# An attention stage and two mixers on one core: the first supergroup by plain weights, and values in longer runs

## The reference, cut to what matters

```python
q_s, k_s = softmax(q, axis=-1), softmax(k, axis=tokens)       # over features; over tokens
x = einsum(q_s, einsum(k_s^T, v))                             # linear attention, (8, 576, 512)
u = x + (relu(x^T @ w_tok1) @ w_tok2)^T                       # token mixing, 576 -> 256 -> 576
y = u + relu(u @ w_ch1) @ w_ch2                               # first mixer,  512 -> 1536 -> 512
out = y + relu(norm(y) * g @ w_ch1') @ w_ch2'                 # second mixer, 512 -> 2048 -> 512
```

## Time and profile before

| | |
|---|---|
| median of 3 runs | 1565.05 us (1563.29 to 1566.54) |
| the profiled execution | 1563.69 us, its span 1561.9 us |
| attention stage | 0 to 243.5 us |
| first mixer, positions 0 to 4 | start at 243.5, 386.9, 501.4, 616.4, 730.0 us |
| second mixer, positions 5 to 9 | start at 844.3, 987.8, 1131.2, 1274.7, 1418.1 us |
| PE, DVE, ACT, POOL busy | 94%, 69%, 45%, 20% of the span |
| mean granted clock | 0.990 |

### The profile page before, as it was taken

How to read it: one execution, slowest core, us unless ns; L and a number is a source line. 1 busy time by engine, 2 the same in 40 slices (tenths; PEclk the granted TensorE clock), 3 DMA queues, 4 the chain that set the end, 5 groups by cost and what they waited for, 6 DMA issues and landing times.

```text
span 1561.9 us, 19837 instructions
## 1 busy us (share of the span) xinstructions
PE 1472.2 (94%) x7584; PEld 1322.4 (85%) x7584; DVE 1076.6 (69%) x1165; ACT 698.2 (45%) x844; POOL 309.0 (20%) x315
## 2 busy tenths in 40 slices
PE   6999896898999999899989999999999999999998
PEld 5988885787888887788878888888888888889998
DVE  7987876397486486496696687568657856872276
ACT  5656654352453453352452453344345424532342
POOL 6587785323303312300000000000000000000000
PEclk9999998899999999999999999999999999999999
DMA  7899985989989989979658767766876687667766
GB/s 241 256 306 296 299 282 202 403 318 366 354 291 379 372 294 362 352 288 317 240 184 300 248 209 266 249 247 219 275 243 228 237 277 244 211 219 256 251 214 199
DMA packets 150334, 429.28 MB, mean 275 GB/s; under 512 B 14240, under 2 KB 43488, under 8 KB 150240
## 3 DMA queue, kind: packets, MB, share of 16 engines
q1 hardware_dynamic: 132768, 361.94, 67.6%
q0 software_dynamic: 17472, 66.07, 11.8%
HBM read 348.26 MB, written 79.69 MB: 274 GB/s over the span
## 4 chain that ended last, share of the span: by engine, by line
PE 74%; DMA 10%; DVE 7%; issue 3%; SPq 2%; POOL 2%; ACT 2%; DVEq 0%; ACTq 0%; POOLq 0%
PE ps L1131 24%; PE ps L1133 23%; PE ps L1132 23%; DMA w_ring<-w_scratch_B 6%; DMA vt<-v 2%; SPq L289 2%; DMA qt<-q 1%; DVE o_lo L980 1%; DVE x_lo L834 1%; PE ps L1155 1%; DMA w_op<-w2b 1%; PE ps L1166 1%; DVE q_sum L761 1%; POOL q_lo L464 0%; DVE h L950 0%
## 5 line engine op out<-in xcount | busy, mean ns | idle before, releaser
L1131 PE MATMUL ps<-x_hi,w_ring 128*128 128x462 f32 (+1 forms) x980 | 369.2, 377 | 44.1 <-issue 15.1
L1131 PE MATMUL ps<-o_hi,w_ring 128*128 128x462 f32 (+1 forms) x980 | 367.4, 375 | 9.6 <-DVE o_lo L980 7.9
L1133 PE MATMUL ps<-x_hi,w_ring 128*128 128x462 f32 (+1 forms) x980 | 366.7, 374 | 0.0
L1132 PE MATMUL ps<-x_lo,w_ring 128*128 128x462 f32 (+1 forms) x980 | 366.7, 374 | 0.0
L1132 PE MATMUL ps<-o_lo,w_ring 128*128 128x462 f32 (+1 forms) x980 | 364.8, 372 | 0.0
L1133 PE MATMUL ps<-o_hi,w_ring 128*128 128x462 f32 (+1 forms) x980 | 364.6, 372 | 0.0
L671 ACT CAST o_hi<-h 128x924 fp32r<-128x924 f32 (+1 forms) x210 | 202.3, 963 | 254.8 <-PE ps L1133 225.0
L980 DVE TENSOR_TENSOR o_lo<-h,o_hi 128x924 fp32r<-128x924 f32 (+1 forms) x210 | 240.8, 1150 | 61.2 <-ACT o_hi L671 61.2
L1131 PEld LDWEIGHTS ps<-x_hi,w_ring 128*128 128x128 f32 x980 | 186.2, 190 | 74.3 <-issue 31.2
L1131 PEld LDWEIGHTS ps<-o_hi,w_ring 128*128 128x128 f32 x980 | 185.1, 189 | 40.1 <-issue 17.5
L950 DVE TENSOR_TENSOR h<-ps,h 128x924 f32<-128x924 f32 (+1 forms) x90 | 100.6, 1117 | 163.5 <-PE ps L1133 163.1
(11 more groups left out here) (140 smaller groups left out, 1831.3 us busy)
## 6 DMA issues: line engine op xcount, KB each, us to landing
w_ring<-w_scratch_C SPq DMA_DIRECT2D x280, 512.0 KB, 3.8
w_ring<-w_scratch_B SPq DMA_DIRECT2D x210, 512.0 KB, 5.6
w_scratch_C<-w_out POOLq DMA_DIRECT2D x8, 1792.0 KB, 11.7
w_scratch_C<-last_pair POOLq DMA_DIRECT2D x8, 1792.0 KB, 11.8
w_scratch_B<-w_out POOLq DMA_DIRECT2D x6, 1792.0 KB, 10.4
w_scratch_B<-last_pair POOLq DMA_DIRECT2D x6, 1792.0 KB, 9.9
kt<-kT SPq DMA_DIRECT2D x32, 288.0 KB, 6.0
u_scratch<-u_out SPq DMA_DIRECT2D x32, 288.0 KB, 3.8
```

Of the source, the lines that this page charges most:

```text
L1131: mm(dst, a_hi, b_hi, start=start, stop=False, skip_group_check=onto)
L1132: mm(dst, a_hi, b_lo, start=False, stop=False, skip_group_check=onto)
L1133: return mm(dst, a_lo, b_hi, start=False, stop=stop, skip_group_check=onto)
```

## The change

Position 0 is no longer a list of ring entries. Its products are plain: for each of 12 units of raw weights (6 of the first matrix, 6 of the second) PE does 48 matmuls of 462 columns, 576 in all, reading the raw blocks from SBUF: slots 0, 5 and 6 of `w_out`, and the fourth block in ring slot 3 (`plain_w`). `CALLS` begins with position 1. The 12 units are all made in this stage: the raw half of a unit first (`hi_raw` on ACT, `lo_raw` on DVE, three instructions each), then the four sums (`sum_unit`, `hi_sums`, `lo_sums`), and its store, which is read from position 1 on. In the attention stage only units 0 and 1 are loaded (batches 5 and 6). POOL makes no remainders of weights any more. `w_out` gets a second buffer of its own. x is split in four parts without sums (`plain_x`), and the hidden blocks in twelve (`hi_po`, `lo_po`). PSUM holds four groups of two banks, which ACT empties with a relu (`plain_take`) after every second unit of the first matrix; `plain_add` adds the last ones into `res`. SP loads x of position 1 and the residual right behind the attention stage, then three ring entries. Units of the second mixer are made at 5 entries in each of positions 1 to 3, unit 12 at the end of position 0.

`vt` becomes [128, 5, 2, 257]: 128 values, one, 128 values, so the ones of two neighbours share a column, and the host lays v out so that four fifths of a batch come in one DMA of runs of 1,024 bytes, with four small ones for the ends and the tail.

```diff
-                for t, rows in ST:
-                    sp.dma_start(vt[0:rows, t, :, 0:P], v[b, t * P:t * P + rows, :].rearrange("p (c e) -> p c e", c=NC))
+                full = vt[:, 0:NT - 1, :, :].rearrange("p t a w -> p (t a w)")
+                w, n = 2 * P + 1, (NT - 1) * NC // 2
+                src = v[b, 0:P * n * 2 * P].rearrange("(p x) -> p x", p=P)
+                sp.dma_start(full[:, P + 1:P + 1 + (n - 1) * w].rearrange("p (n w) -> p n w", w=w)[:, :, 0:2 * P],
+                             src[:, P:P + (n - 1) * 2 * P].rearrange("p (n w) -> p n w", w=2 * P)).then_inc(v_in, 16)
...
             step(NB - 1, 0)
             phase_a_over(sp)
+            for c in range(NC):
+                load_x(1, c)
+            for c in range(NC):
+                load_res(0, c)
+            for n in range(RW - 1):
+                load_entry(n)
+            for c in range(NC):
+                load_x(2, c)
+            store_plain(0)
+            store_plain(1)
+            load_entry(RW - 1)
+            store_plain(2)
+            store_plain(3)
...
-                load_unit(i)
+                if i in (NB - 3, NB - 2):
+                    load_unit(i - (NB - 3))
                 if later:
                     sub_q(i + 1, ST)
-                sum_unit(i - 1)
-                if later:
                     lo_q(i + 1)
-                lo_unit(i - 1)
-                store_unit(i - 1)
+                else:
+                    sum_unit(0)
+                    sum_unit(1)
...
+            for n in range(PLAIN):
+                if n >= 2:
+                    sum_unit(n)
+                store_unit(n)
+                load_unit(n + 2)
...
+            def hi_raw(n):
+                act.wait_ge(wp_in[n % 2], 32 * (n // 2 + 1))
+                wait(act, wp_stored[n % 2], 16 * (n // 2))
+                if n >= 2:
+                    act.wait_ge(groups, unit_over(n - 2))
+                x = w_op[:, n % 2, :, :]
+                nc.scalar.copy(w_out[n % 2][:, 0, 0, :], x[:, 0, :]).then_inc(raw_hi_made, 1)
+                nc.scalar.copy(plain_w(n, 0, 1)[:, 0, :], x[:, 7, :]).then_inc(raw_hi_made, 1)
+                nc.scalar.copy(w_out[n % 2][:, 5:7, 0, :], x[:, 5:7, :]).then_inc(raw_hi_made, 1)
...
+            def plain(n):                                   # ACT
+                if 2 <= n + 1 < PLAIN:
+                    hi_raw(n + 1)
+                if n < HC["B"]:
+                    if n % 2 == 1:
+                        plain_take(n, 0)
+                    hi_sums(n + 1)
+                    if n == 4:
+                        hi_po(0)
+                        hi_po(1)
+                    if n % 2 == 1:
+                        for g in range(1, NC):
+                            plain_take(n, g)
+                    return
...
                 else:                                       # DVE, batches 1 to 7
                     norm_kv(i)
-                    if later == 0:
-                        sum_x(0, 0)
...
+                if later == 0:
+                    lo_raw(1)
+                    lo_px(0)
+                    lo_px(1)
                 if first:
                     max_q(1, ST[3:])
...
+            def plain_in(n):                                # PE, units of the first matrix
+                pe.wait_ge(raw_lo_made, 3 * (n + 1))
+                if n == 0:
+                    pe.wait_ge(px_lo_made, NC)
+                for g in range(NC):
+                    if n == 0 and g == 1:
+                        pe.wait_ge(u_act, U_ACT * NB)
+                        pe.wait_ge(u_dve, U_DVE * NB)
+                    if n >= 2 and n % 2 == 0:
+                        pe.wait_ge(plain_relu, NC * (n // 2 - 1) + g + 1)
+                    for i in range(2):
+                        x = plain_product(plain_w(n, i, g // 2), g % 2, g, *plain_x(2 * i + n % 2),
+                                          n % 2 == 0 and i == 0, n % 2 == 1 and i == 1)
+                    x.then_inc(groups, 1)
```

More of the change, by code:

```diff
@@ L29, in mixer_kernel @@
     CONSTS = 10
+    V_LOADS = 5
     SIZES = [462, 462, 462, 462, 456]
@@ L52, in mixer_kernel @@
     entries = g2_entries = 0
-    for pos in range(NX):
+    for pos in range(1, NX):
         stage, sg = "BC"[pos // NSG], pos % NSG
@@ new lines, in hi_sums, with plain_take, hi_po @@
+            def hi_sums(n):
+                act.wait_ge(wp_sum, 4 * (n + 1))
+                nc.scalar.copy(w_out[n % 2][:, 1:5, 0, :], w_op[:, n % 2, 1:5, :]).then_inc(wp_hi, 1)
+            def plain_take(n, g):
+                act.wait_ge(groups, mixed(n, g))
+                nc.scalar.activation(plain_hidden(g // 2 * HC["B"] + n // 2 * 2 + g % 2), plain_group(g), ACT.Relu)\
+                  .then_inc(plain_relu, 1)
+            def hi_po(r):
+                if r >= RO:
+                    act.wait_ge(groups, added(r - RO))
+                nc.scalar.copy(o_hi[:, r % RO, :, 0:SIZES[0]], plain_hidden(r % 2 * HC["B"] + r // 2)).then_inc(po_hi_made, 1)
@@ L624, in step @@
                             hi_q(i + 1, ST[c - 1:c])
-                    if later == 0 and c == 0:
-                        hi_x(0, 1)
+                    if later == 0 and c < 2:
+                        hi_px(2 + c)
                 if later:
                     hi_q(i + 1, ST[3:])
-                if later and not first:
-                    hi_unit(i - 1)
+                if later == 1:
+                    hi_raw(0)
+                    hi_raw(1)
             exp_q(0, ST)
@@ L691, in norm @@
                       .then_inc(root_made, 1)
-            hi_unit(NB - 2)
-            for p in (2, 3):
-                hi_x(0, p)
-            hi_unit(NB - 1)
+            hi_sums(0)
+            for n in range(PLAIN):
+                plain(n)
             for c in CALLS:
@@ new lines, in plain_add, with plain @@
+            def plain_add(g):
+                n = SIZES[0]
+                y = halves(res, n)[:, g, :, :]
+                if g == 0:
+                    dve.wait_ge(res_in, 64)
+                dve.wait_ge(groups, added(2 * HC["B"] - 1, g))
+                nc.vector.tensor_tensor(y, plain_group(g), y, ALU.add).then_inc(plain_out, 1)
+            def plain(n):
+                if 2 <= n + 1 < PLAIN:
+                    lo_raw(n + 1)
+                if n == 4:
+                    lo_po(0)
+                    lo_po(1)
+                r = 2 * (n - HC["B"]) + 2
+                if 2 <= r < 2 * HC["B"]:
+                    lo_po(r)
+                if n + 1 < PLAIN:
+                    lo_sums(n + 1)
+                else:
+                    lo_unit(PLAIN, 0)
+                    lo_unit(PLAIN, 1)
+                if 2 <= r < 2 * HC["B"]:
+                    lo_po(r + 1)
+                if n == 6:
+                    sum_x(1, 0)
+                if n == 7:
+                    lo_x(1, 0)
+                    lo_x(1, 1)
+                    sum_x(1, 1)
+                if n == 8:
+                    lo_x(1, 2)
+                    sum_x(1, 2)
+                    lo_x(1, 3)
+                if n == 9:
+                    lo_x(1, 4)
+                    lo_x(1, 5)
+                    sum_x(1, 3)
+                if n == 10:
+                    lo_x(1, 6)
@@ L941, in _ @@
             nc.vector.tensor_scalar(g_half[:, :], gcol[:, :], -0.5, None, ALU.mult).then_inc(ghalf_made, 1)
+            lo_sums(0)
+            for n in range(PLAIN):
+                plain(n)
+            for g in range(NC):
+                plain_add(g)
             def take(c, p):
@@ L1339, in tokens_first @@
         return np.ascontiguousarray(a.transpose(0, 2, 1, 3)).reshape(B, S, C)
+    values = tokens_first(inputs["v"])
+    full = values[:, 0:S // 128 * 128]
     arrays = {
@@ L1344 @@
         "kT": np.ascontiguousarray(inputs["k"].transpose(0, 1, 3, 2)).reshape(B, C, S),
-        "v": tokens_first(inputs["v"]),
+        "v": np.concatenate([full.reshape(B, -1, 128, C).transpose(0, 2, 1, 3).reshape(B, -1),
+                             values[:, S // 128 * 128:].reshape(B, -1)], axis=1),
         "w_tok1": np.ascontiguousarray(inputs["moe_w_tok1"]),
```

212 lines of the change are left out of this document (143 added, 69 removed).

## The result

The changed kernel takes **1555.06 us** (median of 6 runs, 1550.73 to 1557.65), the kernel before beside it 1564.17: a ratio of 0.9946, 95% interval 0.9923 to 0.9968. It is faster, by 9 us and not by the 24 of the prediction, and 0.06 us above its range. So the edge of the range says little here; what was missed is a gain of 24 where 9 to 13 came.

The account below looks back on a forecast made before the run. PE, busy 94% of 1561.9 us, bounds the kernel; position 0 is bound by making its own weights. Position 1 starts 24.8 sooner, +1 after it: 1563.7 − 24.8 + 1 = 1539.9, with the median's 1.4 1541 us; range 1530 to 1555.

Parts of the forecast that it names:

- The attention stage, 6.6 us (0 to 13.6): Five attention batches, 144.1 us before, would take 27.5 each, 137.5 in all: a gain of 6.6.
- the storeless batch, 27.6: Attention batch from 60.8 to 88.4 us, in which no unit is stored; used as measure for the five batches.
- Rival 2: Attention stage runs at PE's pace, 7.0 us more gain, and nothing waits after it: 1532 us; chance 0.12.
- It is part of the same 6.6: Values in 1,024-byte runs in the attention stage: their gain is counted inside its 6.6 us, not added.
- The last batch, +1.2 and +0.5: End of the attention stage: added DVE remainders delay the copy of u by 1.2 us, the first product by 0.5 more.
- Position 0, 121.5 + 2 = 123.5: First supergroup: 576 matmuls at 0.211 us are 121.5, plus 2 for all waits, between 0 and 12.
- Rivals 3 and 4: In position 0, unit pairs meeting company cost 19 us (1558, chance 0.06), or stretched sums too cost 52 (1591, chance 0.04).
- the 5 us to spare: Position 0: a unit's chain of 14.6 us is hidden behind 20.2 us of PE work on two units.
- After it. +1, between 0 and 4: From position 1 on: residual additions hidden, a late ring entry, a fifth unit in position 3; together 1 us lost.
- 6 to 8 us for a need 7.6 after it: Start of position 1: ring slot 3's entry, loaded behind the last product and two stores, takes 6 to 8 us.
- Position 1 longer by over 4: Listed sign that the prediction is wrong: position 1 takes over 4 us more than before.
- Rival 5: Attention stage: one long values DMA lands later than short ones, and waits of 9.2 us double: 1555.5; chance 0.03.

Follow-up runs that it names:

- second pair of profiles: The kernel before and the changed kernel, each profiled once more with no further edit: 1564.66 and 1552.96 us, ratio 0.9918 for the changed one.

## Why the prediction was wrong

- **The attention stage, 6.6 us (0 to 13.6): right in kind, too small.** The five batches went from 144.1 to 129.7, a gain of 14.4, beyond even the bound. Two steps failed. The value was taken from the storeless batch, 27.6; but that batch still had a load, its neighbours' transfers and a unit's work. The bound took PE's busy time, 26.1, as a floor; it is none: the batch from 72.8 to 98.3 has PE busy for 25.4 of 25.5 us, and in the whole stage PE's busy time fell from 211.8 to 207.8 us for the same 1,664 matmuls. "DVE is nearly as full as PE" was no bound either: its 24.1 us of a batch would have fitted into 25.5, and in that same batch it is busy for 22.9. Rival 2 (PE's pace) was this part's right answer, at a chance of 0.12.
- **"It is part of the same 6.6" (the values): right, as far as single profiles tell.** The two gains overlap: 14.2 and 4.5 alone, 15.2 together.
- **The last batch, +1.2 and +0.5: the right sign, a third of the size.** The gain of 15.7 us at the last batch's first matmul on `kv` (232.5 to 216.8) became 15.2 at the first product, and 15.0 became 14.4 in the second pair of profiles.
- **Position 0, 121.5 + 2 = 123.5: 127.0 measured** (126.7 again). The price of a matmul held, at 0.210. The one wait stood where the prediction put it, at 20.4 us for unit 2, behind a load of 15.76 (forecast 13 to 18), and took 2.9 for 2. What was left out is the clock behind it (about ten matmuls at half pace, 1.6) and the 1.2 for the residual, said to be hidden. Rivals 3 and 4 did not come: four sums took about 4.0 us in place of 2.9, and the 5 us to spare held.
- **"After it. +1, between 0 and 4": this is the step that failed.** 22.8 us were measured in the first pair of profiles, about 16 over all. The prediction weighed bytes for position 0 ("35.6 MB in 124 us are 287 GB/s, and the kernel moves 343 over 200 us"), where the change takes traffic away, and did not ask it of positions 1 to 3, where it adds. The rows were there: 0.92 of the DMA engines and 338 GB/s in position 1, next to the 343 that it held against the bytes of position 0. "Position 3 gets a fifth unit" was named and given no price; the last quarter of position 3 grew from 26.9 to 29.5 us. The stores of `res` and the ring entry at the seam were priced at "6 to 8 us for a need 7.6 after it"; the entry took 12.0. "Position 1 longer by over 4" was the prediction's own sign of being wrong, and it came.

The errors had opposite signs. The start of position 1 came 6.8 us sooner than forecast (31.6 for 24.8), and the lost 22.8 for 1 turned that into the miss of 14. That the total came so near the range is luck of this kind, and no support for the sum. Rival 5 had nearly the right total, 1555.5, for a reason that did not occur.

What is shown is that PE waits in position 1 for ring entries that take 12 to 15 us, in a stretch where the DMA engines are full, and that the wait follows the late entry when the order changes. How much of the return each transfer at the seam causes stays open. So do why two units fewer in positions 2 and 3 bought nothing, and why the first quarter of position 1 gets shorter (30.7 us) only with the stores spread and the unit at entry 0 gone together, where each of the two alone left it at 35 to 37.

## What to carry to other kernels

A stage that is shortened does not take its transfers with it. Before costing what comes after at nothing, count the DMA issues that now fall into each later stage, and read the DMA share in pieces of 25 us: a mean of 0.92 can be two quarters that are full and one that is at 0.70. Then ask of the piece with DMA to spare what else is full in it, since here it was DVE. And compare the time that a prefetched load takes in the crowd with the time that the ring gives it, here 12 to 15 us against 7.6. PE's busy time is not a floor: here it shrank when the waits went. The count of matmuls times their undisturbed spacing held (576 at 0.210 us in position 0).

## What was not expected of the hardware

- DMA near its limit is slow for everyone in it. From 340 to 380 us, in slices of 1 us, the changed kernel shows this:

```profile
DMA  9930004999999999999999999999998899999999
GB/s 213 389 123 0 0 0 160 241 287 405 421 330 422 381 409 422 360 382 410 422 417 421 420 403 416 411 414 402 408 368 229 282 424 414 426 422 414 434 410 426
```

  Three slices of nothing stand before more than thirty nearly full ones, most of them at 400 to 434 GB/s, in which a 512 KB ring entry takes a median of 15.1 us in place of 6.3. The engines run out of work 10 to 12 us before the seam at which they become the bound. Whether the transfers of the seam could begin in that hole wasn't tried.
- A gap of 5.7 us costs more than 5.7 us: the matmuls behind it come at 0.39 us for a time, at the lower of the two clocks.
- Transfers that nothing waits for lengthened the attention stage by 24 us, the work of as many units by 5, although the DMA share of that stage was 0.71 before they were added.
